# Order of the Vector engine's instructions in the attention slots of a fused RWKV and two-layer feed-forward kernel

## What is computed

```
for t in range(S):
    cur = einsum('bhd,bhe->bhde', u[None] * kt, vt)
    y[:, :, t] = einsum('bhd,bhde->bhe', rt, state + cur)
    state = wt[:, :, :, None] * state + einsum('bhd,bhe->bhde', kt, vt)
x = y as (tokens, 384)
h = x @ w_in;  g = where(h >= 1, h, where(h <= -1, 0, (h + 1)**2 / 4));  x = g @ w_out
h = x @ w2_in; g = where(h > 0, h, exp(min(h, 0)) - 1);                  out = g @ w2_out
```

## Time and profile before

| | us |
|---|---|
| median of 3 timed runs (1011.95 to 1013.45) | 1012.39 |
| the profiled execution's own time | 1013.59 |
| its span, first to last instruction | 1011.4 |
| TensorE busy (97% of the span) | 979.1 |
| Vector engine busy (58%) | 587.4 |
| ScalarE busy (50%) | 502.7 |

### The profile page before, as it was taken

One profiled execution on the slowest core, in us unless ns is written; L12 is line 12 of the kernel. 1 busy time (PEld: TensorE's weight loads), 2 busy tenths in 40 slices (PEclk: granted clock), 3 DMA queues, 4 the chain that ended last, 5 costly groups with the idle time before them and its releaser, 6 DMA issues.

```text
span 1011.4 us, 22395 instructions
## 1 busy us (share of the span) xinstructions
PE 979.1 (97%) x9722; PEld 803.0 (79%) x9722; DVE 587.4 (58%) x919; ACT 502.7 (50%) x895; POOL 48.2 (5%) x44
## 2 busy tenths in 40 slices
PE   8998999999999999999999999999999999999998
PEld 6888987778787778777888888888888888888886
DVE  7788778887779778868543544433333334333332
ACT  4555444454534454444446766554455445444443
POOL 6930000000000000000000000000000000000000
PEclk9999899999999999999999999999999999999999
DMA  8722213122220222020224000000100000000000
GB/s 293 254 97 79 106 34 129 44 79 80 95 80 1 79 95 79 1 80 33 94 70 151 2 30 32 32 32 1 32 31 21 12 32 32 32 1 0 32 1 32
DMA packets 24689, 61.67 MB, mean 61 GB/s; under 512 B 2448, under 2 KB 6928, under 8 KB 24592
## 3 DMA queue, kind: packets, MB, share of 16 engines
q1 hardware_dynamic: 24592, 60.25, 16.8%
HBM read 50.80 MB, written 9.44 MB: 60 GB/s over the span
## 4 chain that ended last, share of the span: by engine, by line
PE 70%; DVE 11%; ACT 1%; issue 1%; ACTq 0%; DVEq 0%
PE down_banks L681 33%; PE work_banks L681 22%; PE first_up_bank L681 15%; DVE g_lo L1390 1%; DVE att L1295 1%; DVE scratch L1414 1%; DVE att L1262 1%; DVE att L1300 1%; DVE att L1306 1%; PE work_banks L796 1%; DVE att L1265 1%; DVE att L1289 1%; DVE att L1267 1%; DVE diagonal L1318 1%; PE work_banks L876 1%
## 5 line engine op out<-in xcount | busy, mean ns | idle before, releaser
L681 PE MATMUL down_banks<-g_hi,wout_lo 128*128 128x512 f32 (+1 forms) x624 | 244.5, 392 | 0.0
L681 PE MATMUL down_banks<-g_lo,wout_hi 128*128 128x512 f32 (+1 forms) x624 | 235.8, 378 | 0.0
L681 PE MATMUL down_banks<-g_hi,wout_hi 128*128 128x512 f32 (+1 forms) x624 | 235.7, 378 | 0.0
L1390 DVE TENSOR_TENSOR g_lo<-scratch,g_hi 128x512 fp32r<-128x512 f32 (+1 forms) x192 | 128.2, 668 | 147.2 <-ACT g_hi L989 147.0
L989 ACT CAST g_hi<-scratch 128x512 fp32r<-128x512 f32 (+1 forms) x192 | 116.0, 604 | 104.6 <-PE down_banks L681 76.6
L1090 ACT ACTIVATE scratch<-first_up_bank,consts 128x512 f32<-128x512 f32 (+1 forms) x88 | 57.2, 650 | 207.4 <-PE first_up_bank L681 207.3
L681 PEld LDWEIGHTS down_banks<-g_hi,wout_lo 128*128 128x128 f32 x624 | 117.7, 189 | 25.6
L681 PEld LDWEIGHTS down_banks<-g_hi,wout_hi 128*128 128x128 f32 x624 | 117.7, 189 | 23.3
L681 PEld LDWEIGHTS down_banks<-g_lo,wout_hi 128*128 128x128 f32 x624 | 118.0, 189 | 21.2
L681 PE MATMUL first_up_bank<-x_hi,win_lo 128*128 128x512 f32 (+1 forms) x336 | 128.2, 382 | 0.3 <-DVE x_lo L1395 0.2
L681 PE MATMUL first_up_bank<-x_hi,win_hi 128*128 128x512 f32 (+1 forms) x336 | 127.5, 380 | 0.0
(11 more groups left out here) (127 smaller groups left out, 1142.4 us busy)
## 6 DMA issues: line engine op xcount, KB each, us to landing
att<-rT_dram SPq DMA_DIRECT2D x12, 512.0 KB, 3.5
att<-kT_dram SPq DMA_DIRECT2D x12, 512.0 KB, 4.4
att<-wT_dram SPq DMA_DIRECT2D x12, 512.0 KB, 5.4
r_nat<-rN_dram SPq DMA_DIRECT2D x12, 384.0 KB, 4.4
k_nat<-kN_dram SPq DMA_DIRECT2D x12, 384.0 KB, 4.2
att<-vN_dram SPq DMA_DIRECT2D x12, 384.0 KB, 5.8
x_dram<-r_nat SPq DMA_DIRECT2D x18, 256.0 KB, 2.3
ynat<-x_dram SPq DMA_DIRECT2D x6, 768.0 KB, 4.2
```

The costliest lines, as they stand in the source:

```text
L681: return nc.tensor.matmul(out, lhsT, rhs, start=start, stop=stop, **kw)
L1390: nc.vector.tensor_tensor(g_of(g_lo, F), sum_of(F), g_of(g_hi, F).bitcast(F32), ALU.subtract).then_inc(glo_ready, 1)
```

## The change

No instruction is added or taken away; the Vector engine's order in slots 32 to 95 is another.

- In `pair_slot` the low part of g and the sum with q move. In levels 0 and 2 they follow the two steps of r; in level 4 they are the last of the slot.
- `ahead_of` no longer has the two suffix products. They are a function of their own, `suffixes`, called in the slot after the double level: first thing, or behind `output` where that slot is a row.
- In the slots without a double level the order becomes: `output` of a row, suffix products, `ahead_of` and `suffixes` for a double level 0 in the next slot, the diagonal part, `update` and `next_decays`, low part of g, the turned x, sum with q, the state.
- The diagonal sums of group 1 move from f = 9 to f = 14.

```diff
--- before.py
+++ after.py
@@ -73,7 +73,7 @@
         8: [("last", 0, 1)], 9: [("turn_k", 0, 1)], 10: [("pair", 1, 0, 0)], 11: [("row_0", 0, 1)],
         12: [("pair", 1, 0, 2)], 13: [("row_1", 0, 1)], 14: [("turn_x", 0, 1)], 15: [("pair", 1, 0, 4)]}
 DIAGONAL = {1: [("values", 1, 1)], 7: [("keys", 2, 0), ("keys", 2, 1)], 8: [("bonus", 2, 0), ("bonus", 2, 1)],
-            9: [("sums", 2, 0), ("sums", 2, 1)], 14: [("values", 2, 0)]}
+            9: [("sums", 2, 0)], 14: [("sums", 2, 1), ("values", 2, 0)]}
 X2_SLOTS = (8, 9, 10)
 WQ = 512
 W2Q = KT * FF // 4
@@ -1264,9 +1264,13 @@
                 dve.wait_ge(ahead_ready[g], done - 1)
                 nc.vector.tensor_tensor(blocks_of(ahead, g, m, 3, 1), blocks_of(ahead, g, m, 2, 1), decays_of(g, m, 1, 1),
                                         ALU.mult).then_inc(ahead_ready[g], 1)
+
+            def suffixes(k, g, l):
+
+                m, done = 2 ** l, ahead_after(k, g, ("pair", l))
+                dve.wait_ge(ahead_ready[g], done)
                 nc.vector.tensor_tensor(single_decays(g, m, 2), single_decays(g, m, 2), single_decays(g, m, 3),
                                         ALU.mult).then_inc(suffix_ready[g], 1)
-                dve.wait_ge(ahead_ready[g], done)
                 dve.wait_ge(suffix_ready[g], done - 1)
                 nc.vector.tensor_tensor(single_decays(g, m, 1), single_decays(g, m, 1), single_decays(g, m, 2),
                                         ALU.mult).then_inc(suffix_ready[g], 1)
@@ -1290,7 +1294,6 @@
                         .then_inc(masked[g], 1)
                 else:
                     nc.vector.copy_predicated(scores[:, :, :, m:4 * m], adjacent_mask, adjacent).then_inc(masked[g], 1)
-                lo_of_g(F - 1)
                 dve.wait_ge(masked[g], scored - 2)
                 nc.vector.copy_predicated(scores[:, :, :, 2 * m:4 * m], apart_mask[:, :, :, 0:2 * m].broadcast_to(shape + [2 * m]),
                                           apart[:, :, :, 0:2 * m]).then_inc(masked[g], 1)
@@ -1299,9 +1302,11 @@
                 dve.wait_ge(masked[g], scored - 1)
                 nc.vector.copy_predicated(scores[:, :, :, 3 * m:4 * m], apart_mask[:, :, :, 2 * m:3 * m].broadcast_to(shape + [m]),
                                           apart[:, :, :, 2 * m:3 * m]).then_inc(masked[g], 1)
-                sum_with_q(F)
                 nc.vector.tensor_tensor(blocks_of(r_, g, m, 2, 2), blocks_of(ahead, g, m, 1, 2, step=2),
                                         decays_of(g, m, 0, 2, same=True), ALU.mult).then_inc(rk_updated[g], 1)
+                if l < 4:
+                    lo_of_g(F - 1)
+                    sum_with_q(F)
                 dve.wait_ge(suffix_ready[g], ahead_after(k, g, stage))
                 nc.vector.tensor_tensor(blocks_of(k_, g, m, 0, 3), blocks_of(k_, g, m, 0, 3), decays_of(g, m, 1, 3),
                                         ALU.mult).then_inc(rk_updated[g], 1)
@@ -1310,6 +1315,9 @@
                                         ALU.mult).then_inc(decay_ready[g], 1)
                 if l < 4:
                     ahead_of(k, g, l + 2)
+                else:
+                    lo_of_g(F - 1)
+                    sum_with_q(F)
 
             def diagonal_sums(k, g):
                 dve.wait_ge(product_ready[g], k + 1)
@@ -1435,32 +1443,44 @@
                     diagonal_part(what, k, g)
                 if F == FIRST[1] - 1:
                     ahead_of(2, 0, 4)
+                    suffixes(2, 0, 4)
 
             def layer1_slot(F):
                 c, f, _ = SLOTS[F]
                 work = work_at(F)
+                before = [what for what, *_ in work_at(F - 1)]
+                for what, k, g, *l in work_at(F - 1):
+                    if what == "pair" and l[0] < 4 and before == ["pair"] and not work[0][0].startswith("row"):
+                        suffixes(k, g, l[0] + 2)
                 if work and work[0][0] == "pair":
                     pair_slot(F, *work[0][1:])
-                else:
-                    lo_of_g(F - 1)
-                    for what, k, g, *_ in work:
-                        if what == "last":
-                            update(k, g, NL - 1)
-                            next_decays(k, g, NL - 1)
-                        if what == "turn_x":
-                            both_x_lo_of(k, g)
-                        if what in ("row_0", "row_1"):
-                            output(k, 2 * g + (what == "row_1"))
-                    sum_with_q(F)
-                    for what, k, g, *_ in work:
-                        if what == "row_1":
-                            next_states(k, g)
-                    if F + 1 < LAYER_1:
-                        for what, k, g, *l in work_at(F + 1):
-                            if what == "pair" and l[0] == 0:
-                                ahead_of(k, g, 0)
+                    for what, k, g in diagonal_at(F):
+                        diagonal_part(what, k, g)
+                    return
+                for what, k, g, *_ in work:
+                    if what in ("row_0", "row_1"):
+                        output(k, 2 * g + (what == "row_1"))
+                for what, k, g, *l in work_at(F - 1):
+                    if what == "pair" and l[0] < 4 and work[0][0].startswith("row"):
+                        suffixes(k, g, l[0] + 2)
+                for what, k, g, *l in work_at(F + 1) if F + 1 < LAYER_1 else ():
+                    if what == "pair" and l[0] == 0:
+                        ahead_of(k, g, 0)
+                        suffixes(k, g, 0)
                 for what, k, g in diagonal_at(F):
                     diagonal_part(what, k, g)
+                for what, k, g, *_ in work:
+                    if what == "last":
+                        update(k, g, NL - 1)
+                        next_decays(k, g, NL - 1)
+                lo_of_g(F - 1)
+                for what, k, g, *_ in work:
+                    if what == "turn_x":
+                        both_x_lo_of(k, g)
+                sum_with_q(F)
+                for what, k, g, *_ in work:
+                    if what == "row_1":
+                        next_states(k, g)
                 if c == NC - 1:
                     w2_lo_of(f - FT)
                     if f in X2_SLOTS:
```

## The result

The changed kernel takes 998.3 us (median of 4 runs, 996.8 to 998.72) where the kernel before takes 1012.17 (4 runs beside it, 1011.54 to 1013.45). The ratio is 0.9852 with a 95% interval of 0.9829 to 0.9875: a gain of 15 us, between 12.7 and 17.3. My forecast was 1000.7, a gain of 11.7, with a range from 998.0 to 1006.5. The sign was right, and so were the waits that were to go; the size was too small, and the ratio puts the time at 0.9852 × 1012.39 = 997.4, 0.6 us under the low end of the range. The median itself lies 0.3 us above that end.

A forecast was written before the change was run, and what follows sets the result against it. TensorE, busy 97% of the span, was taken as the bound, so only its waits could be won. Gains of 2.35, 3.76, 3.80 and 1.83 us in tiles 1 to 4, together 11.7, took 1012.39 to 1000.7; range 998.0 to 1006.5.

The forecast's parts named there:

- The ceiling: Tiles 1 to 4: window length less TensorE's busy time, 14.76 us, is the most any gain can be.
- Double level 4: Eight slots: k ends at W + 4.03 (W: end of the slot's products on TensorE); the 0.88 us wait goes.
- What it exposes: Low part of g comes later: new waits of 0.15 us in slots 55, 71 and 87, 0.45 in all.
- The neighbourhood: Double level 4: the second masked copy directly follows the first, on whose end it waits, costing 0.12 us.
- Double level 0 and the steps ahead: Seven slots and those before: steps ahead fill Vector's 4.23 us idle; waits of 0.58, 1.42 and 0.40 us go.
- Suffix products: Two short ones moved behind the output row: two waits of 0.11 us per tile go; row some 0.7 ahead.
- Diagonal parts: Slots 7, 8 and 14 of the tiles: up to 1.8 us put in front of other Vector work, at cost 0.
- Tile 1's start: Slots 32 to 35: a wait of 0.8 us stays, a new one of 1.0 in slot 34; gain only 0.37.
- B: Rival: margins of 0.19, 0.29 and 0.2 us fail in part, 5.7 us less gain, 1006.4 us; chance 0.15.
- C: Rival: every wait goes, tile 1's included but for 0.52 us in slot 32; 998.2 us; chance 0.05.
- D: Rival: late low part of g in 22 double-level slots, Vector entering each late; slower, 1014 to 1016 us; chance 0.05.
- E: Rival: order freed, but the same wait ends on another engine's next instruction; about 1012 us; chance 0.05.

The follow-up runs named there:

- the third set: The changed kernel once more, with no edit, against the kernel before: 998.83 us against 1011.35, ratio 0.9866.
- the first tile-1 kernel: Changed kernel with slot 33's update first, its diagonal product in slot 35, slot 31's steps ahead before the sum, double level 4 as copy, r, copy, r, copy, k: 997.33 us.

## Why the prediction was right and wrong

**The ceiling was the step that failed.** I took 14.76 us, window less busy time, as all that TensorE can win, and priced each wait at the idle time that its row shows in brackets. Both are short by the same thing. In an unbroken run the next stage starts before the row of the stage ahead has ended: in the fence of slot 48 above, the down matmuls start at 252.67 while the row of the work ends at 252.03 + 0.69 = 252.72. A stage behind up matmuls starts 0.07 us before their row ends, so a wait costs its idle time and 0.07 more. Each kind in tiles 2 to 4 has it, to within two hundredths: idle 0.88 and gain 0.94, 0.40 and 0.47, 0.58 and 0.65, 1.42 and 1.50, 0.12 and 0.19. 24 of the 26 waits went: 24 × 0.07 = 1.7 us, against a shortfall of 13.1 − 11.7 = 1.4. TensorE's busy time of tile 2 fell by 0.3 us though it did the same work, so the recorded lengths hold more than work. The Trainium skill ("Perfetto Trace Analysis", section "Tensor Engine Instruction (MATMUL, LD_WEIGHTS)") says that the profiler estimates a matmul's end from the instruction's size and an SBUF delay and doesn't observe it. That fits these rows; the 0.07 us are their figure, not the page's.

This term alone doesn't carry the time out of the range: 1012.39 − 13.1 = 999.3 is inside it. Of the 3.3 us between the ratio's gain of 15.0 and my 11.7, it is 1.4; 0.4 to 0.6 lie outside the slots at equal clock and have no cause named; the rest, about 1.4, is as much as the clock moves such a figure, which is the next point.

**The range left out the clock.** I wrote that no clock term enters, since the tiles had 1.00. True for the effect in these tiles, not for the times: the kernel before, without any change, has spans from 1007.5 to 1015.5. A difference of 13.5 us at equal clock was measured as 12.5, 13.0 and 13.9 us between medians, and as a ratio of 0.9852. The range needed some 2 us more on either side.

**Double level 4**: right. Forecast, k at W + 4.03 and no wait in slots 48, 64 and 80; k ends at W + 4.06 and there is none. **What it exposes**: 0.15 forecast in slots 55, 71 and 87 and 0.15 to 0.18 measured, and its absence in three kernels shows the cause. That the figure is so close is partly luck: the low part ends at W + 4.88 and not 4.85, and TensorE starts 0.05 behind it and not 0.1. My sign of it, an idle time of 0.15 in tiles 2 to 4, isn't there; only the distance from work to down grew, from 0.57 to 0.72. **The neighbourhood**: forecast 0.12, measured 0.15. **Double level 0 and the steps ahead**: right; all waits of 0.4, 0.6 and 1.4 in tiles 2 to 4 went, and the third copy ends at W + 4.11 (slot 50) where I had 4.08. That Vector is free 2.6 us before the products is what was measured (2.63). **Suffix products**: the small waits went, and the split is part of the cause; the 0.7 us of margin that I gave the row was too much, some 0.6 of delay used it up. **Diagonal parts**: nearly right; slot 40 lost 0.12, which I had at nothing. **Tile 1's start**: 0.8 in slot 33 (0.81 shown), 1.0 in slot 34 (0.80 shown, 0.87 with the 0.07), 0.25 in slot 35 (0.36 from start to start). The kernel with the update in front shows that the order in slot 33 is the cause.

**The rivals.** B didn't come about. C, all waits gone, would have been right about the time (998.2) and wrong about the reason: tile 1's waits are there. D was not what happened; that a late low part costs, and more than its waits where the clock falls behind them, the kernel with the low part last shows. E fell: no wait passed to another engine in slots 32 to 95.

What I left unsaid in the prediction, and should have drawn from my own sums: each half of the change needs the other for its full worth. The experiments show it, 0.1 and 8.4 against 13.1.

## What to carry to other kernels

Where one engine is the bound and its queue is never empty, a wait is found by the place of one instruction in another engine's queue: write down when the consumer arrives and when each candidate ends, and the order falls out; in tiles 2 to 4 it did so here to a tenth of a microsecond. Put work that waits for nothing into the hole in front of an instruction that waits for another engine, and only then push the low-priority work back. Here the first alone gave 8.4 us, the second alone 0.1, as it only moved the waits, and both 13.1. Price a wait from start to start against the same stage without a wait, not from the idle time that the row shows, and compare executions at equal granted clock when a per cent matters.

## What the runs showed of the hardware

**A stall of 2 to 3 us can cost twice.** In the kernel before, TensorE waits 2.09 us at about 100 us, in slots that the change doesn't touch, and was busy 3.70 and 3.47 us of the two stretches of 5 us around it. The granted clock in them and after:

```profile
95.00:100.00 5.00, 3.70 (x96) 3.26 (x95) 4.97 (x7) 1.31 (x4) 0.00 (x0) 1.00 0.01 3
100.00:105.00 5.00, 3.47 (x82) 3.34 (x83) 3.08 (x6) 0.62 (x2) 0.00 (x0) 0.61 0.28 82
105.00:110.00 5.00, 5.00 (x33) 5.00 (x33) 2.49 (x8) 1.92 (x5) 0.00 (x0) 0.70 0.00 0
```

The same stretches of the changed kernel's profile:

```profile
95.00:100.00 5.00, 3.94 (x99) 3.50 (x97) 4.96 (x8) 1.29 (x3) 0.00 (x0) 1.00 0.00 0
100.00:105.00 5.00, 3.23 (x93) 3.17 (x94) 3.87 (x7) 0.85 (x3) 0.00 (x0) 1.00 0.27 82
105.00:110.00 5.00, 4.85 (x96) 4.50 (x95) 4.36 (x10) 3.47 (x9) 0.00 (x0) 1.00 0.02 3
```

The same work, as many idle microseconds, and in one execution the clock falls to the lower level (1.2 GHz) for part of the time, in the other it stays at 2.4 GHz. It isn't the kernel: the profile of the third set is of the changed kernel too, and there the clock falls.

```profile
105.00:110.00 5.00, 5.00 (x35) 5.00 (x34) 2.91 (x9) 2.32 (x6) 0.00 (x0) 0.76 0.00 0
```

Up to there the two kernels are equal, so that difference of 2.2 us in the profiles is no effect of the change. The kernel with the low part last shows the fall in close view: after an idle 2.79 us the matmuls run 1.3 us at 0.23 us from start to start, then 3.4 us at 0.43, then at 0.23 again. It happened after three of its seven long waits. Of six executions of that kernel four had a mean clock of 0.989, the lowest of the study.

**One execution ran at half speed throughout.** The profiled execution of the first tile-1 kernel has a span of 1913.1 us. Its down matmuls:

```profile
519.73 0.61 PE L681 MATMUL down_banks<-g_lo,wout_hi 128*128 128x512 f32 x1
520.17 0.61 PE L681 MATMUL down_banks<-g_hi,wout_hi 128*128 128x512 f32 x1
520.62 0.72 PE L681 MATMUL down_banks<-g_hi,wout_lo 128*128 128x512 f32 x1
521.07 0.71 PE L681 MATMUL down_banks<-g_lo,wout_hi 128*128 128x512 f32 x1
```

They start 0.45 us apart, where they start 0.23 apart in the others, and TensorE waits for another engine once, 1.5 us, while the granted clock of the record reads 1.000. The five other executions of the kernel took 994.8 to 999.1 us. Nothing in the runs tells why. The granted clock of a record was therefore not enough here to know the speed of an execution; the distance between two matmuls showed it.
